# Top-k attention, softplus MLP and routed experts on one core: new instruction orders in the first ten steps and behind attention, weights split one unit of each projection a step, the low part behind the first strikes

## The reference

```
scores = q @ k^T / 8                       # 4 batches x 8 heads, 576 x 576, head dim 64
kth    = 32nd largest score of each row
attn   = softmax(where(scores >= kth, scores, -1e9))
x      = attn @ v                          # -> 2304 tokens x 512
h      = x @ w_in                          # 512 x 2048
x2     = softplus(h) @ w_out               # 2048 x 512; softplus = relu(h) + log1p(exp(-|h|))
logits = x2 @ w_gate                       # 8 experts; each token takes its best one
out    = gate * (relu(x2 @ w1[e]) @ w2[e]) # w1: 512 x 1024, w2: 1024 x 512
```

## Time and profile before

| | us |
|---|---|
| median of 3 runs (lowest, highest) | 1138.36 (1137.43, 1139.7) |
| profiled execution | 1137.76 |
| its span | 1136.0 |
| PE busy | 1016.1 (89%) |
| DVE busy | 841.6 (74%) |
| ACT busy | 723.4 (64%) |
| POOL busy | 715.3 (63%) |
| mean granted clock of PE | 0.956 |

### The profile page before, as it was taken

How to read it: one execution, slowest core, us unless ns; L and a number is a source line. 1 busy time by engine, 2 the same in 40 slices (tenths; PEclk the granted TensorE clock), 3 DMA queues, 4 the chain that set the end, 5 groups by cost and what they waited for, 6 DMA issues and landing times.

```text
span 1136.0 us, 21411 instructions
## 1 busy us (share of the span) xinstructions
PE 1016.1 (89%) x6951; PEld 814.2 (72%) x6952; DVE 841.6 (74%) x1848; ACT 723.4 (64%) x1337; POOL 715.3 (63%) x624
## 2 busy tenths in 40 slices
PE   3555699999999999999999999999998999999976
PEld 1333477787777777777778777777797778888864
DVE  7777899999999999999999999998063722222241
ACT  3666688888788788788788888788645111111130
POOL 3666688888888888888887888888543212211101
PEclk9855699999999999999999999999999999999989
DMA  9650025353234353233263333233365141111100
GB/s 337 246 208 1 1 75 165 106 173 112 75 130 148 125 159 123 75 130 112 75 214 106 123 130 112 75 130 112 124 223 191 51 182 39 55 37 37 46 9 18
DMA packets 38477, 130.46 MB, mean 115 GB/s; under 512 B 4016, under 2 KB 13232, under 8 KB 27632
## 3 DMA queue, kind: packets, MB, share of 16 engines
q1 hardware_dynamic: 35344, 119.57, 29.8%
q0 software_dynamic: 3040, 9.70, 2.6%
HBM read 111.43 MB, written 18.09 MB: 114 GB/s over the span
## 4 chain that ended last, share of the span: by engine, by line
PE 38%; POOL 37%; issue 10%; ACT 10%; DVE 2%; DMA 2%; SPq 1%; DVEq 0%; ACTq 0%; POOLq 0%
POOL pr L1385 14%; POOL pr L1388 7%; PE psum L655 6%; PE psum L656 6%; PE psum L657 6%; POOL h_lo L1399 5%; POOL hs L1393 5%; PE psum L524 3%; ACT h_hi L855 3%; POOL pr L1381 3%; PE psum L542 3%; PE psum L603 2%; PE psum L582 2%; PE psum L584 1%; PE psum L583 1%
## 5 line engine op out<-in xcount | busy, mean ns | idle before, releaser
L1046 DVE MAX8 top<-work 128x8 f32<-128x576 f32 x432 | 306.3, 755 | 0.0
L1385 POOL TENSOR_SCALAR pr<-sc,top 128x576 f32<-128x576 f32 x96 | 213.6, 2225 | 9.6
L1052 DVE MATCH_REPLACE8 work<-top,work 128x576 f32<-128x576 f32 x288 | 212.8, 751 | 0.0
L524 PE MATMUL psum<-ident,pr 128*128 128x128 f32 (+1 forms) x720 | 114.8, 294 | 75.0 <-ACT pr L816 63.3
L563 PE MATMUL psum<-x_parts,wi_hi 128*128 128x256 f32 x576 | 169.7, 295 | 1.7 <-DVE x_parts L1058 1.6
L564 PE MATMUL psum<-x_parts,wi_hi 128*128 128x256 f32 x576 | 162.8, 283 | 0.0
L565 PE MATMUL psum<-x_parts,wi_lo 128*128 128x256 f32 x576 | 162.6, 282 | 0.0
L524 PEld LDWEIGHTS psum<-ident,pr 128*128 128x128 f32 (+1 forms) x720 | 79.7, 143 | 111.1 <-ACT pr L816 73.7
L810 ACT ACTIVATE pr<-pr,bias 128x576 f32<-128x576 f32 x144 | 111.7, 776 | 68.2 <-POOL pr L1388 65.9
L1393 POOL TENSOR_TENSOR hs<-hs,ab 128x512 f32<-128x512 f32 x72 | 92.0, 1277 | 81.1 <-ACT ab L847 81.1
L1388 POOL TENSOR_TENSOR pr<-pr,sc 128x576 f32<-128x576 f32 x96 | 136.7, 1424 | 8.0
(11 more groups left out here) (193 smaller groups left out, 2078.2 us busy)
## 6 DMA issues: line engine op xcount, KB each, us to landing
wo_ring<-wo_parts SPq DMA_DIRECT2D x72, 1024.0 KB, 4.8
wo_parts<-wo_ring SPq DMA_DIRECT2D x8, 1024.0 KB, 4.0
kT<-in_k SPq DMA_DIRECT2D x16, 288.0 KB, 3.5
qT<-in_q SPq DMA_DIRECT2D x16, 288.0 KB, 4.4
vtok<-in_v SPq DMA_DIRECT2D x16, 256.0 KB, 2.9
wo_raw<-in_moe_w_out SPq DMA_DIRECT2D x1, 4096.0 KB, 14.8
wi_raw<-in_moe_w_in SPq DMA_DIRECT2D x1, 4096.0 KB, 25.0
x_rows<-x2tok SPq DMA_DIRECT2D x16, 256.0 KB, 2.6
```

The costliest lines, as they stand in the source:

```text
L524: mm = nc.tensor.transpose(transit[0:keys, c, :], pr[:, n % 2 * 2 + t, c * P:c * P + keys], ident[:])
L1046: nc.vector.max(top[:, at, 8 * r:8 * r + 8], sc[:, at, :] if r == 0 else work[:, t, :]).then_inc(topk_step, 1)
L1052: nc.vector.match_replace(work[:, t, :], top[:, at, 8 * r - 8:8 * r], sc[:, at, :] if r == 1 else work[:, t, :], TAKEN).then_inc(topk_step, 1)
L1385: nc.gpsimd.tensor_scalar(to, sc[:, at, :], top[:, at, TOPK - 1:TOPK], OUT, ALU.is_lt, ALU.mult).then_inc(mask_step, 1)
```

## The change

- The raw and the split w_in are laid out by unit, and w_in is loaded by four transfers (one for each 128 rows) whose runs in SBUF are 1 KB. From step 1 on, each step splits one unit of w_out, from step 2 on one unit of w_in; POOL makes the low part of a w_in unit one step after ACT's high part.
- ACT has a written-out order of its own for the steps before MLP_AT; in the middle `normalise` stands ahead of `cut_off`.
- DVE does `x_low(n - 3)` behind the strikes of round 1. Up to block 9 it does `reciprocals(n - 1)` at the end of block n; later `reciprocals(n - 2)` stays behind the maxima of round 0.
- Behind attention: PE turns token tiles 14 and 15 inside `up(LASTG, 1)`, does their logits ahead of `last_down(0)`, the early count behind it, and `slots_early` ahead of `up(LASTG, 5)`; `slots_late` moves into the first `e_down`. DVE makes the gates behind the star, splits both halves of w2 ahead of the last `choose`, and does `relu(1)` and `h_low(1)` later. SP loads the star's weights further ahead of the w_out units. w1 of the star is split in quarters on ACT and DVE. POOL gathers the first two tiles behind `h_low` of units 4 and 5 (before: behind units 6 and 7).

```diff
-def wo_units(i):
-    return range(2 * (i - 1), 2 * i) if 1 <= i <= UNITS // 2 else ()
-def wi_units(i):
-    return wo_units(i - UNITS // 2)
+def wo_unit(i):
+    return i - 1 if 0 <= i - 1 < UNITS else None
+def wi_unit(i):
+    return wo_unit(i - 1)
...
     phase("gap_b", [P, WLEN - 4 * PAIRS * SEQ // 2 - PAIRS * (FULL + 1) * P - 6 * TOPK - 3 * 8])
-    wi_hi = phase("wi_hi", [P, KD, FF], F32R)
-    wi_lo = phase("wi_lo", [P, KD, FF], F32R)
+    wi_hi = phase("wi_hi", [P, UNITS, KD, 2 * P], F32R)
+    wi_lo = phase("wi_lo", [P, UNITS, KD, 2 * P], F32R)
...
         sp.dma_start(wo_raw[:], w_out.rearrange("(k p) n -> p k n", p=P)).then_inc(wo_loaded, 16)
-        sp.dma_start(wi_raw[:], w_in.rearrange("(k p) f -> p k f", p=P)).then_inc(wi_loaded, 16)
+        for kk in range(KD):
+            sp.dma_start(wi_raw[:, :, kk, :], w_in[kk * P:(kk + 1) * P, :].rearrange(
+                "p (u f) -> p u f", u=UNITS)).then_inc(wi_loaded, 16)
...
                     load_v(PLAN[n][1] + 1, p)
-            for u in wo_units(i):
-                store_wo(u)
+            if wo_unit(i) is not None:
+                store_wo(wo_unit(i))
...
             store_piece(2 * (LASTG - 1) + a)
-        for u in range(2, 4):
-            load_wo(first + u)
+        load_wo(first + 2)
...
         w2_to = wbuf[:, 0, KD * EF:].rearrange("p (k n) -> p k n", k=KE)
-        for u in range(4, 8):
-            for n in ((0, 1) if u < 6 else ()):
-                at = slice((u - 4) * 512, (u - 3) * 512)
-                half = slice(n * KD // 2, (n + 1) * KD // 2)
-                sp.dma_start(w1_to[:, half, at], w1_from[:, half, at]
-                             ).then_inc(w1_first if u == 4 else w1_loaded[0], 16)
-            for n in ((0, 1) if u >= 6 else ()):
-                at = slice((2 * (u - 6) + n) * KE // 4, (2 * (u - 6) + n + 1) * KE // 4)
-                sp.dma_start(w2_to[:, at, :], w2_from[:, at, :]
-                             ).then_inc(w2_first if u == 6 else w2_loaded[0], 16)
+        def load_first(c):
+            for n in range(2):
+                if c < 2:
+                    at, half = slice(c * 512, (c + 1) * 512), slice(n * KD // 2, (n + 1) * KD // 2)
+                    sp.dma_start(w1_to[:, half, at], w1_from[:, half, at]
+                                 ).then_inc(w1_loaded[0] if c else w1_first, 16)
+                else:
+                    at = slice((2 * (c - 2) + n) * KE // 4, (2 * (c - 2) + n + 1) * KE // 4)
+                    sp.dma_start(w2_to[:, at, :], w2_from[:, at, :]
+                                 ).then_inc(w2_loaded[0] if c > 2 else w2_first, 16)
+        load_first(0)
+        load_wo(first + 3)
+        load_first(1)
+        load_first(2)
+        load_wo(first + 4)
+        load_first(3)
+        for u in range(5, 8):
...
             if halves:
-                pe.wait_ge(first_split, 1)
+                pe.wait_ge(quarter_split, 2)
...
                 if n and halves:
+                    pe.wait_ge(quarter_split, 3)
...
             down(LASTG - 1, UNITS - 1, part)
-        up(LASTG, 1)
-        turn_tokens(LASTG - 1, NT - 4, 0)
-        turn_tokens(LASTG - 1, NT - 3, 1)
-        last_down(0)
+        up(LASTG, 1, {(1, 0): lambda: turn_tokens(LASTG - 1, NT - 4, 0),
+                      (1, 2): lambda: turn_tokens(LASTG - 1, NT - 3, 1)})
...
+        last_down(0)
+        count_early()
...
-        count_early()
...
+        slots_early()
         up(LASTG, 5)
-        slots_early()
...
         e_up(1, rank_first)
-        e_down(0, 0, rank_first, {KE // 2: lambda: turn_h(1)}, halves=True)
-        slots_late()
+        e_down(0, 0, rank_first, {KE // 2: slots_late, KE // 2 + 1: lambda: turn_h(1)}, halves=True)
...
         def split_wi(u):
-            act.wait_ge(wi_loaded, 16)
-            act.wait_ge(wo_split, UNITS)
-            nc.scalar.copy(wi_hi[:, :, u * 2 * P:(u + 1) * 2 * P],
-                           wi_raw[:, :, u * 2 * P:(u + 1) * 2 * P]).then_inc(wi_hi_ready, 1)
+            act.wait_ge(wi_loaded, 16 * KD)
+            act.wait_ge(wo_split, u + 1)
+            nc.scalar.copy(wi_hi[:, u], wi_raw[:, u]).then_inc(wi_hi_ready, 1)
...
             now, late = is_block(i - 1), is_block(i - 2)
+            if i < MLP_AT:
+                if late:
+                    normalise(i - 2, 0)
+                    normalise(i - 2, 1)
+                if now:
+                    for t in cuts(i - 1):
+                        cut_off(i - 1, t)
+                scores_out(i + AHEAD, 0)
+                scores_out(i + AHEAD, 1)
+                if late:
+                    probs_out(i - 2, 0)
+                if wo_unit(i) is not None:
+                    split_wo(wo_unit(i))
+                if now:
+                    exponentials(i - 1, 0)
+                if late:
+                    probs_out(i - 2, 1)
+                if now:
+                    exponentials(i - 1, 1)
+                if wi_unit(i) is not None:
+                    split_wi(wi_unit(i))
+                if late:
+                    x_out(i - 2)
+                continue
...
+            if late:
+                normalise(i - 2, 0)
+                normalise(i - 2, 1)
...
-            if late:
-                normalise(i - 2, 0)
-                normalise(i - 2, 1)
...
                 exponentials(i - 1, 1)
-            for u in wo_units(i):
-                split_wo(u)
-            for u in wi_units(i):
-                split_wi(u)
...
         turn_out(NT - 3, 1)
-        up_out(1)
+        rectify(LASTG, 1)
...
+        logarithm(LASTG, 1)
+        h_high(LASTG, 1)
+        gate_exps(0)
         up_out(2)
-        gate_exps(0)
-        up_out(3)
-        up_out(4)
-        up_out(5)
-        first_w1(0)
-        up_out(6)
-        first_w1(1)
+        for u in range(3, 7):
+            up_out(u)
+            first_w1((u - 3) // 2, (u - 3) % 2)
...
+        first_w2(1)
...
-        first_w2(1)
...
                         strike(n, t, r)
+                if r == (1 if is_block(n) else 0) and is_block(n - 3):
+                    x_low(n - 3)
...
-                if r == 0 and is_block(n - 3):
-                    x_low(n - 3)
-                if r == 0 and is_block(n - 2):
+                if r == 0 and n > MLP_AT and is_block(n - 2):
                     reciprocals(n - 2)
+            if 0 < n < MLP_AT:
+                reciprocals(n - 1)
...
         choose(SOME, 0)
-        gates(SOME, 0)
...
         nc.vector.tensor_copy(eid_i[:], eid[:]).then_inc(star_ready, 1)
+        gates(SOME, 0)
...
         h_low(0)
-        first_w2(1)
-        relu(1)
...
+        relu(1)
...
         nc.vector.tensor_copy(rank_i[:, EARLY:NTAB], rank_e[:, EARLY:NTAB]).then_inc(tiles_ready, 1)
-        h_low(1)
...
         nc.vector.tensor_copy(dst_i[:, MAIN], dstf[:, MAIN]).then_inc(tables_ready, 1)
+        h_low(1)
...
                     mask(i - 1, t)
-            for u in wo_units(i):
-                low_wo(u)
-            for u in wi_units(i):
-                low_wi(u)
+            if wi_unit(i - 1) is not None:
+                low_wi(wi_unit(i - 1))
+            if wo_unit(i) is not None:
+                low_wo(wo_unit(i))
...
-        for u in range(UNITS - 1):
+        for u in range(5):
...
         pool.wait_ge(tables_ready, 1)
-        gather(0, 0, TOK - 2 * P)
+        for T in range(EARLY):
+            gather(T, T, TOK - 2 * P)
+            softplus(LASTG, 5 + T)
+            h_low(LASTG, 5 + T)
...
-        gather(1, 1, TOK - 2 * P)
```

More of the change, by code:

```diff
@@ L174, in build @@
         wo_raw = phase("wo_raw", [P, KF, DM])
-        wi_raw = phase("wi_raw", [P, KD, FF])
+        wi_raw = phase("wi_raw", [P, UNITS, KD, 2 * P])
         scope.close()
@@ L265, in build @@
         first_hi, first_split = sem("first_hi"), sem("first_split")
+        quarter_hi, quarter_split = sem("quarter_hi"), sem("quarter_split")
         xs_split, e_h_split = sem("xs_split"), sem("e_h_split")
@@ L545, in times_v, with up @@
                 mm.then_inc(pv_ready, 1)
-            def up(g, u):
+            def up(g, u, amid=()):
                 n = UNITS * g + u
@@ L558, in up @@
                 for part in range(2):
-                    f = slice((2 * u + part) * P, (2 * u + part + 1) * P)
+                    f = slice(part * P, (part + 1) * P)
                     for kk in range(KD):
+                        if (part, kk) in amid:
+                            amid[part, kk]()
                         first, last = kk == 0, kk == KD - 1
                         hi, lo = x_parts[:, g % 2, 0, kk, :], x_parts[:, g % 2, 1, kk, :]
-                        nc.tensor.matmul(ps[:, part, :], wi_hi[:, kk, f], hi, start=first, stop=False)
-                        nc.tensor.matmul(ps[:, part, :], wi_hi[:, kk, f], lo, start=False, stop=False)
-                        mm = nc.tensor.matmul(ps[:, part, :], wi_lo[:, kk, f], hi,
+                        nc.tensor.matmul(ps[:, part, :], wi_hi[:, u, kk, f], hi, start=first, stop=False)
```

(35 more changed lines are left out.)

6 lines of the change are left out of this document (2 added, 4 removed).

## The result

The changed kernel takes 1127.14 us in the median (1125.37 to 1128.85, 4 runs) against 1137.89 us (1136.92 to 1139.70, 4 runs) beside it: 0.9904 of the time, 95% interval 0.9883 to 0.9924. The gain is 10.7 us where 23 were forecast; the range just missed it. The profiled execution took 1126.6 us, its span was 1124.9, so the two traces lie 11.1 us apart, much as the medians do. The granted clock is PE's, as a share of 2.4 GHz: 1.00 is that level, 0.50 is 1.2 GHz, and a value between them is a stretch with both. A hole is a stretch in which PE sits idle.

What follows compares the result with a forecast made beforehand. A loop of waits was taken to bound the first steps, PE the part behind attention. Gains of 20.5 - 0.3 + 3.3 = 23.5 us off the profiled 1137.76 gave 1114.3, as a median 1115; range 1107 to 1127.

Steps and rivals of the forecast that it cites:

- the 13.17 us: First steps: time of a later block before the change, said to be set by a loop of waits, every engine having slack.
- The start's price: First blocks: block 2 starts at 28.3 us instead of 26.77, 1.5 us lost, and block 3 at 38.3.
- that term: First steps: w_in in 1 KB runs lands at 38 us and costs nothing; upper bound 2 us.
- PE's first transposes wait for the low part: First steps: low part done at T+3.1 after DVE's block start T; DVE then bounds a block at 10.15 us.
- rival (a): First steps still close through ACT; at 11.7 us a step or w_in 4 us late, 12 us less gain: 1127; chance 0.10.
- the term: Start and transition into the middle: a gain of 20.5 us, with softplus of the first unit at 122.0 instead of 141.87.
- Middle: Middle groups: the later low part costs seven groups 0.3 us in all, up to 12 if uncovered, -3 if time feeds back.
- Rival (b): Middle: the later low part is not covered at unit 0, 7 x 1.7 = 12 us lost, 1127; chance 0.07.
- rival (c): Middle: low part gates PE's transposes in all 62 steps, slower than before from 0.38 us a step, 1145; chance 0.04.
- The last low part and the gather: Behind attention: with POOL's gather moved earlier, the last softplus starts about 862.5 and the last low part ends 1.6 us sooner.
- The clock: Behind attention: PE's hole shrinks from 3.5 to 2 us; if the clock stays up, 1.7 us gained, half counted: 0.9.
- The late slots: First expert product: late slots inside it and w2's second split moved remove PE's 0.56 us wait and a little more: 0.8.

Runs made afterwards that it cites:

- e2: The changed kernel with ACT copying the scores out ahead of the cut in the first ten steps: 1122.19 us, ratio 0.9848 to the kernel before.
- e11: The changed kernel with ten unread transposes of the identity in each of steps 2 to 9: 1122.83 us, ratio 0.9850 to the kernel before.
- e4: The changed kernel with DVE's x_low behind the first maxima again, ahead of the strikes: 1125.05 us, ratio 0.9874 to the kernel before.
- e5: The changed kernel with the late slot tables behind the first e_down and h_low(1) ahead of the tables, both as before: 1125.92 us, ratio 0.9881.
- e3: The changed kernel with only the late slot tables put back behind the first e_down: 1129.64 us, ratio 0.9917 to the kernel before.
- e10: e8 with ten unread transposes of the identity in each of steps 2 to 9: 1114.26 us, ratio 0.9784 to the kernel before.
- e8: e7 with POOL's first gather behind h_low(5) and the second behind the last h_low: 1112.37 us, ratio 0.9779 to the kernel before.
- e7: The changed kernel with scores copied ahead of the cut, x_low behind the first maxima, and everything behind attention as before: 1115.87 us, ratio 0.9802.
- e1: The changed kernel with everything behind attention as before: 1125.44 us, ratio 0.9875 to the kernel before.
- e9: e7 with 16 unread transposes of the identity ahead of PE's wait for the first gathered tile: 1115.59 us, ratio 0.9802 to the kernel before.

## Why the prediction was right and wrong

**The bound now and the start: right, as far as tested.** That the 13.17 us were a loop and not a full engine is shown: from step 2 on the changed kernel too splits two weight units a step, in another order, and with one more edit (e2) a block takes 10.09. So it was the order, not the number of units; no run puts the old order of the splits back alone. The start's price (block 2 at 28.13, block 3 at 38.02) came out within 0.3 us. w_out took 14.6 us to land, and ACT waited 4.99 us for it, which the forecast had priced; w_in landed at about 37.5, and ACT waited 0.23 us, so that term was rightly nothing. Its runs of 1 KB went at about 348 GB/s (27 to 35 us), w_out's at 386 (15 to 19 us): the measurement decides against the rule by which w_in would have landed at 36.

**The failed step in the first steps** is "PE's first transposes wait for the low part". They wait for ACT's copy of the scores, which the changed order puts 2.8 us behind x out. I had listed the orders of ACT and the waits of the low part, and not every semaphore at the head of `turn_probs`. Forecast: transposes from T+3.1, 10.15 us a block. Measured: a loop of 11.33 through ACT and PE, 10.88 in the mean, block 10 4.8 us late. e2 takes that gate away and gives 10.09: the bound was right, the gate was missed. It was rival (a) in kind (the steps close through ACT), though not by that rival's reason: its price of 11.7 is 1.55 us above DVE's bound, the measured mean 0.73. The loop has PE's transposes and products in it, and e11, where they run at a higher clock, has it shorter. Part of the 4.8 us came back at the transition (softplus 4.2 late, block 10's reciprocals 3.6 short of the term).

**Middle: a term too small.** The wait for x_parts at unit 0 grew to 1.72 to 1.79 us in five of seven groups (forecast about 1.9), and it was covered in most: 1.7 us lost in all, forecast 0.3; e4 puts about 2 us on the later low part. Rival (b)'s mechanism acted in part, rival (c) did not: its 0.38 us a step would have been seen in every block.

**The failed steps behind attention, the largest miss: 4.1 lost instead of 3.3 gained.** Each of the three terms failed in the profiled execution.
- The last low part and the gather (1.6): the first gather did move away from the last softplus, but this softplus then waits 2.09 us for ACT's logarithm. Counted from group 8's first up-projection, that logarithm starts at 51.3 us, 1.0 later than before, because the last up-projection is later: PE waits 0.22 and 0.63 us for earlier low parts ahead of it, and behind it 0.34 and then 1.92 for the last. Ahead of the 0.63, one softplus took 2.31 us instead of 1.28 beside DVE's one-hot table at 821.5 to 823.8. The Trainium skill, "SBUF — State Buffer", Who interferes with whom, has DVE and GpSimd share a pair of ports under an exclusive lock; this row agrees. The collision isn't new: in the kernel before, the same DVE instruction (at 844.50) goes with a low part of 2.85 us, for which PE doesn't wait. In all, the last down starts only 0.2 us sooner behind group 8's first up-projection.
- The clock (0.9): 0.64 again, so nothing in this trace. Six traces have this code with a last wait of 1.83 to 1.92 us: the clock fell in four (the changed kernel, e2, e5, e11) and stayed at 1.00 in two (e3, e4), where the stretch takes 1.6 us less. Counting half of the 1.7 us was fair, and 1.6 of the 4.1 us is the luck of this execution.
- The late slots (0.8): the sign was wrong. In the kernel before, the tables (2.11 us of PE, from 894.80) stood between the two products while ACT and DVE made the second tile's hidden halves. ACT's copy can't start until the first product is done, as both tiles use one buffer: it starts at 882.10 in the changed kernel and at 895.06 before, right behind that product in both. With the tables inside the product nothing covers it; the wait went from 0.56 to 2.51. I had taken the idle time before an instruction for the cost of what stood next to it, not asked what covered it.
- 2.3 us more went in the clock behind the holes of 6.32 and 2.66 us at the end, a place that I had called untouched; e5 gets it back with the late slots, and why is open.

## What to carry to other kernels

Before forecasting an order, list every semaphore at the head of the moved instruction and of each instruction that waits for it, and where the new order puts each of the signals; one missed gate cost 4.9 us here, and moving two lines gave it back. When work is moved out of a place between a producer and its consumer, ask what it was covering. And undo tests must undo all edits that share a queue, or they show the other edit (e3).

## What the runs showed of the hardware

- The length of the last hole doesn't tell whether the granted clock falls. The same code behind the same wait (1.92 us) ran at 0.63 in the changed kernel and at 1.00 in e4, and e10 fell to 0.50 with no hole just ahead, where e8 stayed at 1.00. At the end of the kernel it does go with the order. Behind the same two holes (6.32 and 2.66 us) the stretches of 10 and 5 us ran at 0.70 and 0.69 in the changed kernel and at 0.79 and 1.00 in e5. The five traced kernels with the long wait at the second product down (2.51 to 2.65 us: the changed one, e2, e3, e4, e11) took 234.0 to 234.2 us from the second tile's output to the end, the other seven 231.7 to 232.1. Why a wait 190 us earlier goes with it is open.
- The same code started at different paces: e7 and e8 have the same first steps, and in the profiles a block took 10.64 us in one and 10.1 in the other. In the first PE's opening transposes took 1.30 us, at the lower clock, in the second 0.74. Block 10's reciprocals came at 137.0 to 139.6 us in four traces of one first stage (the changed kernel, e1, e3, e5) and at 131.5 to 134.3 in three of another (e7, e8, e9). A difference of up to 3 us between the starts of two profiles shows nothing by itself.
- Work that nobody reads can pay: fillers in PE's idle time gained 4 to 6 us where PE was in the loop (e11), and nothing where it wasn't (e10).
